# Spectral filter and top-1 mixture of experts: the second batch brought back and routed in two halves, the first expert block started before the last batch is back

## The reference

```python
X = np.fft.rfft(x, axis=1)
y = np.fft.irfft(X * (filt_r + 1j * filt_i)[None], n=3072, axis=1)
x = y.reshape(8 * 3072, 256)                      # in the expert part, N = 3072 gives cap = 3072 // 8 * 2 = 768
logits = x @ w_gate                               # 8 experts
expert_idx = np.argmax(logits, axis=1)
gate_w = softmax(logits)[arange, expert_idx]
# in token order: token i takes the next free slot of its expert, if it has fewer than 768
h = np.maximum(disp[e] @ w1[e], 0)                # 768 x 256 @ 256 x 1024
y = h @ w2[e]                                     # 768 x 1024 @ 1024 x 256
out[i] = gate_w[i] * y[expert_idx[i], pos[i]]     # zero where a token has no slot
```

## Time and profile before

| | us |
|---|---|
| median of 3 runs | 542.0 (539.07, 542.0, 543.35) |
| the profiled execution: its own time | 540.95 |
| its span, first to last instruction | 539.1 |
| busy PE / PE weight loads / DVE / ACT / POOL | 470.7 / 376.3 / 221.7 / 206.6 / 216.8 |
| granted TensorE clock, mean of the span | 0.970 |
| PE's share of the chain that ended last | 66% |

### The profile page before, as it was taken

The page is one execution under the profiler, slowest core; times in us unless marked ns, Lnnn a source line. Parts: engine busy times, 40 slices in busy tenths (PEclk is TensorE's granted clock), DMA queues, the critical chain, the costliest instruction groups (busy, mean ns, idle before and its releaser), DMA issues.

```text
span 539.1 us, 9489 instructions
## 1 busy us (share of the span) xinstructions
PE 470.7 (87%) x3806; PEld 376.3 (70%) x3806; DVE 221.7 (41%) x335; ACT 206.6 (38%) x362; POOL 216.8 (40%) x190
## 2 busy tenths in 40 slices
PE   5446787999979877988988998999999999998993
PEld 2114333355535444487987998999999999997993
DVE  7025114333354789478626323245322444223210
ACT  2301333455535514534135534344542445433320
POOL 7080110000000000747355788655867657584222
PEclk9959889999999999989999999999999999999997
DMA  8989999998678394999623119941199230771001
GB/s 291 339 296 407 406 380 311 301 339 295 199 253 317 111 301 123 366 406 394 235 69 117 60 23 390 330 136 33 35 368 358 65 114 29 254 298 37 30 32 34
DMA packets 64534, 119.73 MB, mean 222 GB/s; under 512 B 7760, under 2 KB 35296, under 8 KB 64480
## 3 DMA queue, kind: packets, MB, share of 16 engines
q1 hardware_dynamic: 38912, 76.39, 40.0%
q0 software_dynamic: 9824, 25.33, 13.0%
q10 hardware_dynamic: 15744, 17.31, 9.5%
HBM read 60.78 MB, written 58.23 MB: 221 GB/s over the span
## 4 chain that ended last, share of the span: by engine, by line
PE 66%; DMA 11%; DVE 8%; issue 6%; ACT 4%; SPq 2%; ACTq 1%; POOL 0%; POOLq 0%; DVEq 0%
PE back L1320 21%; PE wide L1306 11%; PE bank L1306 11%; PE back L520 7%; PE low L553 4%; PE low L535 4%; DMA u_scratch<-v_out 3%; PE wide L507 3%; DVE pq L828 2%; PE low L688 2%; PE bank L568 2%; ACT v_out L720 2%; DMA w_raw<-in_w 2%; DMA t_scratch<-t_out 2%; SPq L405 1%
## 5 line engine op out<-in xcount | busy, mean ns | idle before, releaser
L1320 PE MATMUL back<-w2h,hh 128*128 128x256 f32 x384 | 109.8, 286 | 0.0
L1320 PE MATMUL back<-w2h,hl 128*128 128x256 f32 x384 | 108.6, 283 | 0.0
L1320 PE MATMUL back<-w2l,hh 128*128 128x256 f32 x384 | 108.6, 283 | 0.0
L828 DVE TENSOR_TENSOR pq<-wide,fab 128x1024 f32<-128x1024 f32 x45 | 55.0, 1223 | 112.2 <-PE wide L507 108.8
L1131 DVE SCALAR_TENSOR_TENSOR hl<-wide,hh 128x384 fp32r<-128x384 f32 x64 | 34.6, 555 | 120.5 <-ACT hh L1083 78.6
L1220 POOL DMA_INDIRECT out<-o_out,token x48 | 50.1, 1043 | 83.0 <-ACT o_out L1092 62.8
L1320 PEld LDWEIGHTS back<-w2h,hh 128*128 128x128 f32 x384 | 73.6, 192 | 0.2 <-issue 0.2
L1320 PEld LDWEIGHTS back<-w2l,hh 128*128 128x128 f32 x384 | 73.6, 192 | 0.0
L1320 PEld LDWEIGHTS back<-w2h,hl 128*128 128x128 f32 x384 | 73.6, 192 | 0.0
L1192 POOL DMA_INDIRECT g_in<-y_rows,token x48 | 52.9, 1103 | 33.1 <-DVE token L999 17.4
L1092 ACT ACTIVATE o_out<-back,o_gate 128x256 f32<-128x256 f32 x48 | 22.9, 477 | 101.8 <-PE back L1320 94.6
(11 more groups left out here) (131 smaller groups left out, 790.4 us busy)
## 6 DMA issues: line engine op xcount, KB each, us to landing
out<-zero SPq DMA_DIRECT2D x24, 1024.0 KB
w_raw<-in_w SPq DMA_DIRECT2D x14, 1024.0 KB
u_scratch<-v_out ACTq DMA_DIRECT2D x48, 192.0 KB, 4.2
z_in<-t_scratch SPq DMA_DIRECT2D x24, 256.0 KB, 4.4
x_in<-in_x POOLq DMA_DIRECT2D x12, 512.0 KB, 13.6
t_scratch<-t_out ACTq DMA_DIRECT2D x15, 256.0 KB, 6.6
t_scratch<-t_out SPq DMA_DIRECT2D x15, 256.0 KB, 5.6
x_in<-in_x SPq DMA_DIRECT2D x6, 512.0 KB, 6.1
```

The costliest lines, as they stand in the source:

```text
L828: nc.vector.tensor_tensor(pq[:, n % 3], spectrum(t, h)[:, :, 0, :].unsqueeze(2).to_broadcast([P, 2, 2, D]), fab[:, h], ALU.mult).then_inc( ...
L1320: mm = nc.tensor.matmul(ps[4 + (b * ST + s) % 2][:, 0:D], hx[:, b % 2, f, s * P:(s + 1) * P], wt[:, k, f, :], start=(f == 0 and m == 0), s ...
```

## The change

Token batches and stages are now numbered apart: token batch 0 is the first batch, 1 and 2 are the first and second half of the second batch (stage 1), and `LATE` = 3 is the half of the third (stage 2). `halved(b)` is true of 1, 2 and 3: 6 products each, of two matmuls of 64 rows, 12 columns in every routing step, 12 table matmuls instead of 24, exponentials of half width.

- The last stage has functions of its own in the first round (`*_halves_stage`). Tokens of half 1 run in steps 3 to 5, three at a time, those of half 2 in steps 6 to 10. The route of batch 0 is denser (`FULL_STEPS`), that of half 1 runs in steps 7 to 9 (`EARLY_STEPS`) with its table in step 9, and the first 22 steps of that of half 2 in steps 11 and 12 (`HALF_STEPS`).
- SP loads the chunks in the order 0, 3, 1, then a z load, then 4, 2, 5, as half a batch takes columns of both; the z loads and y stores behind are interleaved anew.
- The tokens of blocks 0 and 1 come from batch 0 and half 1 alone. POOL gathers block 0 within the stage (into `g_first`), the casts and the w1 low part of expert 0 move into it too, and its turn stands before the last inverse product, into the banks of `wide`.
- After the stage: `up` of block 0 takes the place of the 10 unused matmuls; between its groups DVE does the rest of half 2's route (`LATE_ROUTE`); then the table of half 2, the tokens of `LATE`, the turn of block 1. POOL splits w2 of expert 0 when up 0 has ended; w2 of expert 1 is split by DVE instead of POOL.
- In `pe_experts` the order is then up 1, down 0, table of `LATE`, and on as before. `pool_experts` and `sp_last`'s order (chunks, weights of expert 1, y stores, nine zero writes) are as before.

```diff
-UNUSED = 10
 LAST_STEPS = [0, 0, 0, 4, 8, 12, 20, 23, 26, 28, 30, 30, 30, 30, 30, 30]
 NEXT_STEPS = [0, 0, 0, 0, 0, 0, 0, 0, 0, 0, 3, 6, 8, 10, 14, 18]
-FIRST_ROUTE = [4, 8, 9, 10, 10, 12, 12, 13, 14]
-NEXT_ROUTE = [14, 15, 16, 17, 18, 20, 22, 22, ONE_HOT + 6]
+NEXT_ROUTE = [4, 8, 8, 10, 10, 16, 20, 22, ONE_HOT + 6]
+LATE_ROUTE = [22, 23, 23, 24, 24, 25, 26, 27, 28]
+HALVES = [[], [], [], [(1, 0), (1, 1), (1, 2)], [(1, 3), (1, 4), (1, 5)], [(1, 6), (1, 7), (1, 8)], [(2, 0), (2, 1)],
+          [(2, 2), (2, 3)], [(2, 4), (2, 5)], [(2, 6), (2, 7)], [(2, 8)], [], [], [], [], []]
+FULL_STEPS = [0, 0, 4, 10, 22, 24, 28, 30, 30, 30, 30, 30, 30, 30, 30, 30]
+EARLY_STEPS = [0, 0, 0, 0, 0, 0, 0, 10, 25, 30, 30, 30, 30, 30, 30, 30]
+HALF_STEPS = [0, 0, 0, 0, 0, 0, 0, 0, 0, 0, 0, 10, 22, 22, 22, 22]
+FULL_TABLE = 7
+EARLY_TABLE = 9
+FULL_RANK = 4
+EARLY_RANK = 8
+HALF_RANK = 12
...
+            if r == 0:
+                for c in (0, 3, 1):
+                    v_chunk(sp, ai, c)
+                z_load(sp, t, ZB)
+                for c in (4, 2, 5):
+                    v_chunk(sp, ai, c)
+                sp.dma_start(tri_half[:, :], tri_d).then_inc(half_set, 16)
+                z_load(sp, t, ZB + 1)
+                y_store(sp, 1, 0)
+                y_store(sp, 1, 1)
+                z_load(sp, t, ZB + 2)
+                y_store(sp, 1, 2)
+                z_load(sp, t, ZB + 3)
+                y_store(sp, 2, 0)
+                z_load(sp, t, ZB + 4)
+                sp.wait_ge(ya_done, ya_before(2) + 4)
+                sp.nop(nofuse=True)
+                raw_load(sp, r, 0, 0)
+                raw_load(sp, r, 0, 1)
+                y_store(sp, 2, 1)
+                y_store(sp, 2, 2)
+                return
             for c in range(3):
                 v_chunk(sp, ai, c)
...
+        def pe_halves_stage(pe, t, r):
+            for h in range(NH):
+                pe_forward(pe, t, r, h)
+                if NH + h < AI_FROM + span(0):
+                    pe_tokens(pe, 0, NH + h - AI_FROM, t + 1, False)
+                if h == FULL_RANK:
+                    pe_rank(pe, 0, 7)
+                for b, i in HALVES[h]:
+                    ranked = 0 if b == 1 else 1 if i > 4 else None
+                    pe_tokens(pe, b, i, t + 1, False, ranked)
+                    if h == EARLY_RANK and i == 4:
+                        pe_rank(pe, 1, 7)
+                    if h == FULL_TABLE and i == 2:
+                        pe.wait_ge(v_evac, t * NG + h // 2)
+                        pe_table(pe, 0, 4)
+                if h == EARLY_TABLE:
+                    pe.wait_ge(v_evac, t * NG + h // 2)
+                    pe_table(pe, 1, 4)
+                if h == HALF_RANK:
+                    pe_rank(pe, 2, 7)
+                if h == FULL_TABLE + 1:
+                    pe.wait_ge(route_step, ROUTE_STEPS)
+                if h == EARLY_TABLE + 1:
+                    pe.wait_ge(route_step, 2 * ROUTE_STEPS)
+                if h >= 2 and h % 2 == 0:
+                    pe_inverse(pe, t, h // 2 - 1)
+            pe.wait_ge(m_done, t * NH + NH - 1)
+            pe_block_turn(pe, r, 0)
+            pe_inverse(pe, t, NG - 1)
+
...
         def pe_last(pe, t, r):
-            pe.wait_ge(v_evac, (t + 1) * NG)
             if r == 0:
-                pe.wait_ge(m_done, (t + 1) * NH)
-                for _ in range(UNUSED):
-                    nc.tensor.matmul(ps[2][:, 0:3 * P], ident, sq[:, :, :], start=True, stop=True)
-            pe_table(pe, t - 1, 4)
-            for i in range(span(t)):
-                pe_tokens(pe, t, i, t + 1, True, t - 1)
-                if r == 0 and i == products(t):
-                    pe_block_turn(pe, r, 0)
+                pe_up(pe, r, 0, None)
+                pe.wait_ge(v_evac, (t + 1) * NG)
+                pe_table(pe, 2, 4)
+                for i in range(span(LATE)):
+                    if i == 1:
+                        pe.wait_ge(hl_done, FT)
+                    pe_tokens(pe, LATE, i, t + 1, True, 2)
+                    if i == products(LATE):
+                        pe_block_turn(pe, r, 1)
...
+        def act_halves_stage(act, t, r):
+            for h in range(NH):
+                if h == FULL_EXP:
+                    act_exp(act, 0)
+                if h == EARLY_EXP:
+                    act_exp(act, 1)
+                if h == HALF_EXP:
+                    act_exp(act, 2)
+                if NH + h < AI_FROM + span(0):
+                    act_tokens(act, 0, NH + h - AI_FROM, False, True)
+                for b, i in HALVES[h]:
+                    act_tokens(act, b, i, False, False)
+                if h >= 2 and h % 2 == 0:
+                    act_back(act, t, h // 2 - 1)
+                if h == FIRST_W1:
+                    act_split(act, r, 0, 0, t + 1)
+                if h == FIRST_W2:
+                    act_split(act, r, 0, 1, t + 1)
+            act.wait_ge(bi_done, (t + 1) * NG - 1)
+            act_block_turned(act, r, 0)
+            act_back(act, t, NG - 1)
+
...
+        def dve_halves_stage(dve, t, r):
+            for h in range(NH):
+                dve_multiply(dve, t, r, h)
+                before = h - 1 if h else 0
+                dve_steps(dve, 0, FULL_STEPS[before], FULL_STEPS[h])
+                dve_steps(dve, 1, EARLY_STEPS[before], EARLY_STEPS[h])
+                if h == EARLY_TABLE:
+                    dve_tokens(dve, 1, 0)
+                    nc.vector.tensor_scalar(least[:, 1:2], least[:, 0:1], 2.0, None, ALU.mult).then_inc(flag_set, 1)
+                if h == FIRST_W1L:
+                    dve.wait_ge(m_done, t * NH + h + 1)
+                    low_split(dve, r, 0, 0)
+                dve_steps(dve, 2, HALF_STEPS[before], HALF_STEPS[h])
+            dve.wait_ge(bi_done, (t + 1) * NG)
+            dve_block_turned(dve, r, 0)
+
...
         def dve_last(dve, t, r):
-            for n in range(NEXT_STEPS[-1], HOT):
-                dve_route(dve, t - 1, n, 7)
-            for n in range(HOT, ROUTE_STEPS):
-                dve_route(dve, t - 1, n, 4)
+            b = token_batch(t)
             if r == 0:
-                dve_tokens(dve, t - 1, 0)
-                nc.vector.tensor_scalar(least[:, 1:2], least[:, 0:1], 2.0, None, ALU.mult).then_inc(flag_set, 1)
-            low_split(dve, r, 0, 0)
-            if r == 0:
-                dve.wait_ge(bi_done, (t + 1) * NG)
+                for f in range(FT):
+                    dve_upped(dve, r, 0, f)
+                    dve_steps(dve, 2, LATE_ROUTE[f], LATE_ROUTE[f + 1])
                 nc.vector.memset(zero[:, :], 0.0).then_inc(zero_set, 1)
+                dve_steps(dve, 2, HOT, ROUTE_STEPS)
+            else:
+                for n in range(NEXT_STEPS[-1], HOT):
+                    dve_route(dve, b - 1, n, 7)
+                dve_steps(dve, b - 1, HOT, ROUTE_STEPS)
+                low_split(dve, r, 0, 0)
...
-            if e < 2:
+            if r == 0 and e == 0:
+
+                act.wait_ge(m_done, (last - 1) * NH + (10 if w else 2))
...
-                                          (w2h, w2l, w2h_done, w2l_done, "p j d -> p (j d)", nc.gpsimd))[w]
+                                          (w2h, w2l, w2h_done, w2l_done, "p j d -> p (j d)",
+                                           nc.vector if (r, e) == (0, 1) else nc.gpsimd))[w]
...
         def pool_last(pool, t, r):
-            gate_store(pool, t - 1)
             if r == 0:
+                gate_store(pool, 1)
                 pool.wait_ge(set_up, SET_UP)
+                pool.wait_ge(tokens_set, 3)
+                rows_ready(pool, 2)
+                pool.wait_ge(ya_done, ya_before(LATE))
+                pool_gather(pool, r, 0)
+                gate_store(pool, 2)
                 pool.wait_ge(bi_done, (t + 1) * NG)
-                pool.wait_ge(tokens_set, 3)
-                rows_ready(pool, t)
-                pool_gather(pool, r, 0)
+                pool_gather(pool, r, 1)
+                pool_after(pool, r, 0, FT)
+                pool.wait_ge(m_done, (t + 1) * NH)
                 low_split(pool, r, 0, 1)
-                pool_gather(pool, r, 1)
-                pool_after(pool, r, 0, 5)
                 pool_gates(pool, r, 0)
-                low_split(pool, r, 1, 1)
-                gate_store(pool, t)
+                gate_store(pool, LATE)
+                pool_after(pool, r, 1, 3)
                 pool_gates(pool, r, 1)
```

More of the change, by code:

```diff
@@ L80, in batch_of, with token_batch, stage_of, halved @@
     return t if t < FIRST else t - 1
-def products(t):
-    return N2 // 4 if t == HALF else N2 // 2
+def token_batch(t):
+    return t if t < HALF else t + 1
+def stage_of(b):
+    return b if b < HALF else b - 1
+def halved(b):
+    return HALF - 1 <= b <= LATE
+def first_row(b):
+    return A1 if b == HALF else 0
+def products(b):
+    return N2 // 4 if halved(b) else N2 // 2
 def ya_before(t):
@@ L98, in gates_before @@
 def gates_before(t):
-    return 16 * sum(2 if k == HALF else 1 for k in range(t))
```

(66 more changed lines are left out.)

307 lines of the change are left out of this document (171 added, 136 removed).

## The result

The change makes the kernel slower: **563.7 us** (561.11 to 564.93, 4 runs) against 541.7 (4 runs), a ratio of **1.038, 95% interval 1.033 to 1.044**. I had forecast 551 and a range of 541 to 558: the direction holds, the size doesn't. The profiled execution took 563.83 us, span 562.0, clock 0.938 (before 540.95, 539.1, 0.970).

What follows compares the result with a forecast made beforehand. PE was taken as full from slice 24 on, the loss lying in the first half: the last stage, its wait and the first expert blocks. 540.95 + 10.3 (stage) - 1.1 (behind it) + 1.0 (clock) = 551 us, range 541 to 558.

Steps and rivals of the forecast that it cites:

- the stage: Third (last) stage, up to the end of the last inverse product: that end comes 10.3 us later, bounds +3 and +12.
- Up to forward 6: First part of the last stage: late chunks 2.5, added tail 2.6 and 0.7 more bring this product to 174.9.
- Forward 4: Forward product early in the last stage, expected near 163, with PE losing 2.5 us to late chunks (bounds 0.8 and 4).
- From forward 6 to S: Rest of the last stage, to the end of the last inverse product: +4.5 us, DVE working without holes of its own.
- holes in steps 8 to 15: DVE in the last stage: it was to run without holes from step 7; idle gaps here would prove the forecast wrong.
- Rival E: Thin tail of the stage: clock falls, up 0 runs at half speed, 8.3 us more, 559 us; chance 0.14.
- Products at S+16.9: Last batch's first product, 16.9 us behind the last inverse product's end (formerly 9.7); POOL's w2l holds two DVE steps.
- rival B: Behind the stage: POOL's w2l holds no DVE step, 5.9 us gained before the turn of block 2, 545.8 us; chance 0.11.
- The zeros: Nine 1 MB writes before POOL's sends: 26.6 us long, setting the turn of block 2, leaving 1.1 us gained.
- Rival C: Behind the stage: zero writes land early, the chain over tokens decides, 8.9 us gained, 542.4 us; chance 0.12.
- The low clock behind: Behind the turn of block 2, after PE stands about 9 us: slow clock costs 0 to 1.7 us, taken as 1.
- Rival D: Last stage: DVE's idle 17.6 us absorb the second route, its end stays, 8.9 us come off, 532 us; chance 0.13.

Runs made afterwards that it cites:

- experiment 7: Kernel before with half batch's routing on 12 columns: 0.993, again 0.996; plus block 2 gathered first: 1.014; half routing plus w2l of expert 1 on DVE (last fence): 0.999.

## Why the prediction was wrong

- **The step that failed is the stage: +10.3 forecast, +17.0 and +15.5 measured.** The mechanism, more work and later loads in front of S, is right; its size isn't. I had two parts of it. Up to forward 6 I forecast +5.8; it is +9.4 and +8.2. Forward 4, which I had near 163, 17.1 behind forward 0, came at 19.3 and 18.3: the two late chunks cost 1.2 to 2.2 more than the 2.5 that I took between 0.8 and 4, and the third product waits for the second of them even at full clock. From forward 6 to S I forecast +4.5; it is +7.6 and +7.2. There I added up DVE's work and said "in order and without a hole of its own". Its work was right, 35.2 against 35.4, but I gave it 2.6 us of waits and gaps and it had 5.9: PE's queue holds the rank product ahead of a ready inverse, and DVE's multiplies wait for the forwards behind it. That coupling is shown for the stretch from multiply 11 on (17.3 to 14.2); S gained only 0.4 to 1.6 from its removal, so it is not shown to be the whole 3 us. Of the sum for forward 6, the 0.7 at its end stands there without a source, and the way from forward 4 to forward 6 took 13.3 where it leaves 11.9. I had named holes in steps 8 to 15 as what would make the forecast wrong.
- **Rival E**, the clock, had the condition right and the price wrong. The clock did fall, to 0.66 in 160 to 170 and 0.79 in 210 to 220. Filling the waits restored it and gave nothing back. Up 0 itself ran at the full level; it had no 8.3 us to lose.
- **Products at S+16.9: S+16.8.** Part of that is luck: I let both hot_hi steps wait for w2l, but only the second did, and w2l took 5.12 instead of 4.57. The hold by POOL's w2l is shown for a bfloat16 step of two SBUF operands: 4.58 beside it, 0.75 without. My rival B is out. The Trainium skill ("SBUF — State Buffer", its section on the two separate sides) has the pair of ports as an exclusive lock; by that rule the step waits whatever its data type, and the trace agrees: 4.58.
- **The zeros**: they bound the turn, as forecast. From their issue (258.75) to POOL's release (288.56) it took 29.8 us instead of 26.6, so the send came at S+59.4 instead of S+55.4, and the turn at S+68.9 instead of S+64.8. The sign of that term turned: +2.9 and +1.3 instead of -1.1. Rival C is out by the same row.
- **The low clock behind**, +1.0, is the turn's 1.54 instead of 0.88 and little more.
- **Ahead of the stage** I forecast nothing; 3.1 to 5.7 were lost, part of it the scatter of executions. It was in no term of mine.
- **Rival D** needed DVE's 17.6 idle us. S did not stay: the last multiply came at 227.2. From 156.4 to the end of multiply 6 DVE is idle for 14.2 of 29.7 us in the changed kernel too, in front of most of the new work, as I argued.

Term by term against 22.9: 5.7 ahead of the stage, 17.0 in it, 2.9 behind S, -2.7 at the end. Mine were 0, 10.3, -0.1, 0. Not settled: why multiply 11 starts 0.6 to 2.0 us behind the modelled end of its forward in ten of the eleven profiles (the rows name no other releaser than PE or "remote"), and what of the 3 us ahead of the stage is the change's.

## What to carry to other kernels

Work that is pulled into a stage in front of its bottleneck can cost more than its duration if it puts an item into an in-order queue that waits for another engine: price the queue behind the item, not the item. A low clock in a wait is a symptom; before you price it, ask what the next instruction would have waited for at full speed. Of a change with several parts, time the part that only removes work alone: here it was the one gain. And follow a gain to S and to the end: 3.1 us won in one stretch were 0.4 to 1.6 at S and nothing in the time.

## What the runs showed of the hardware

- The hold between POOL and DVE goes both ways. A DVE subtraction of two SBUF operands (2.28 us) beside it stretched POOL's issue of an indirect DMA from 1.0 to 3.09 us (last fence of experiment 7). The kernels before and after show it with w1l, also 2.28 or 2.29 long: gathers of 2.22 (from 218.35) and 2.55 (from 300.18) before, 2.43 (from 327.14) after. All four end 0.87 to 0.95 behind the end of the DVE instruction, nearly the 1.0 that an issue takes by itself: it is held until DVE is done.
- Nine zero writes of 1 MB took 29.8 us from the first issue to the release of POOL, at a DMA share of 1.01 to 1.03 and 347 to 374 GB/s in the windows from 260 to 290.
- The kernel before took 541.7 us in the first timing, 547.5 to 547.9 on three chips and 553.3 on one more. No chip on record was timed at two different times, so chip and time are not told apart; a difference between two kernels is read only from runs made side by side on one chip.
